# The delta-rule attention's TensorE program without its loop, and the output product in two halves of the array

## The reference: what is computed

```python
k_n = k / (np.linalg.norm(k, axis=-1, keepdims=True) + 1e-06)
state = np.zeros((B, H, D, D), dtype=np.float32)
for t in range(S):
    kt, vt, bt = (k_n[:, :, t], v[:, :, t], beta[:, :, t, None])
    y[:, :, t] = np.einsum('bhd,bhde->bhe', q[:, :, t], state)
    v_old = np.einsum('bhde,bhd->bhe', state, kt)
    state = state + bt[:, :, :, None] * np.einsum('bhd,bhe->bhde', kt, vt - v_old)
```

## Time and profile before

| | us |
|---|---|
| median of three runs | 1100.64 (1093.97, 1100.64, 1100.87) |
| profiled execution: its own time | 1103.74 |
| profiled execution: span | 1102.0 |
| of it, first to last output product of the attention | 66.8 to 396.5 |
| TensorE busy in the span | 967.5 (88%) |
| VectorE | 630.4 (57%) |
| ScalarE | 586.7 (53%) |
| GpSimd | 259.2 (24%) |

### The profile page before, as it was taken

The page is one execution under the profiler, slowest core; times in us unless marked ns, Lnnn a source line. Parts: engine busy times, 40 slices in busy tenths (PEclk is TensorE's granted clock), DMA queues, the critical chain, the costliest instruction groups (busy, mean ns, idle before and its releaser), DMA issues. The chain is left out here.

```text
span 1102.0 us, 25678 instructions
## 1 busy us (share of the span) xinstructions
PE 967.5 (88%) x10563; PEld 673.8 (61%) x10563; DVE 630.4 (57%) x1106; ACT 586.7 (53%) x1141; POOL 259.2 (24%) x303
## 2 busy tenths in 40 slices
PE   1798998989899884069999999999999999999996
PEld 0587887878788752046666667655555555555553
DVE  5678686868678546356665654244444444444442
ACT  2566574747477552346666664354545454454542
POOL 6556463646256111710000000000101001010101
PEclk9989897979799977589999999999999999999998
DMA  6022132312122001774555541000000000000000
GB/s 215 16 81 86 43 102 66 91 55 77 43 69 63 2 1 53 241 252 145 150 155 151 151 155 47 1 1 1 29 1 29 1 1 29 0 29 0 29 1 29
DMA packets 38108, 74.05 MB, mean 67 GB/s; under 512 B 3817, under 2 KB 29553, under 8 KB 38001
## 3 DMA queue, kind: packets, MB, share of 16 engines
q1 hardware_dynamic: 34928, 63.05, 18.5%
q0 software_dynamic: 3072, 9.45, 2.3%
HBM read 63.04 MB, written 9.45 MB: 66 GB/s over the span
## 5 line engine op out<-in xcount | busy, mean ns | idle before, releaser
L1406 PE MATMUL bankH<-rows_or_y,wd 128*128 128x512 f16 (+1 forms) x864 | 201.8, 379 | 1.6 <-PEq L1045 1.6
L1418 PE MATMUL bankO<-wd,gd_hi 128*128 128x384 f16 x768 | 187.4, 326 | 0.6
L1406 PEld LDWEIGHTS bankH<-rows_or_y,wd 128*128 128x128 f16 x864 | 84.5, 98 | 93.5 <-issue 1.7
L665 DVE CAST_PREDICATED merge<-pair_mask,bankA 128x512 f16<-128x512 uint16 x144 | 100.5, 698 | 56.1 <-PE bankA L346 55.9
L1418 PE MATMUL bankO<-wd,gd_lo 128*128 128x384 f16 x384 | 125.2, 326 | 0.0
L534 ACT CAST x_inv<-bankA 128x512 f16<-128x512 f32 x120 | 70.4, 587 | 86.2 <-PE bankA L357 86.2
L1418 PEld LDWEIGHTS bankO<-wd,gd_hi 128*128 128x128 f16 x768 | 74.6, 98 | 62.1 <-DVE gd_lo L1480 2.8
L1503 POOL DMA_INDIRECT out<-o_rows,dest x24 | 25.6, 1069 | 346.7 <-ACT o_rows L1457 290.4
L1473 DVE SCALAR_TENSOR_TENSOR gd<-hd_exp,hd 128x512 f32<-128x512 f32 x96 | 66.5, 692 | 66.8 <-ACT hd_exp L1443 66.8
L1480 DVE SCALAR_TENSOR_TENSOR gd_lo<-gd,gd_hi 128x512 f16<-128x512 f32 x96 | 66.5, 692 | 64.4 <-ACT gd_hi L1451 64.4
L1451 ACT ACTIVATE gd_hi<-gd 128x512 f16<-128x512 f32 x96 | 60.4, 630 | 69.1 <-DVE gd L1473 69.0
(11 more groups left out here) (187 smaller groups left out, 1791.5 us busy)
## 6 DMA issues: line engine op xcount, KB each, us to landing
kq_t<-in_kq_rows SPq DMA_DIRECT2D x24, 512.0 KB, 4.6
stage<-in_moe_w SPq DMA_DIRECT2D x24, 512.0 KB, 3.6
stage<-in_moe_w SPq DMA_DIRECT2D x32, 384.0 KB, 3.6
rows_or_y<-x_sorted SPq DMA_DIRECT2D x12, 385.0 KB, 7.4
k_norm<-in_k_tok SPq DMA_DIRECT2D x24, 192.0 KB, 2.4
v_in<-in_v_tok SPq DMA_DIRECT2D x24, 192.0 KB, 2.4
k_tok<-in_k_tok SPq DMA_DIRECT2D x24, 192.0 KB, 3.5
stage<-in_moe_w_in SPq DMA_DIRECT2D x8, 384.0 KB, 3.2
```

What stands on the lines that cost most here:

```text
L665: nc.vector.copy_predicated(half_cols(merge[:, i], i, False), pair_mask[:, i, :].rearrange("p (n b) -> p n b", b=2 << i).unsqueeze(1) .to_ ...
L1406: last = nc.tensor.matmul(h_bank[f % 4][:, :], wd1[:, a, c, P * f:P * f + P], y_t[:, b, c, bass.ds(blk * NB, NB)], start=c == a == b == 0, ...
L1418: last = nc.tensor.matmul(o_bank[s][:, 0:DM], (g_lo if a else g_hi)[:, f % 4, P * s:P * s + P], wd2[:, b, f, :], start=f == a == b == 0, s ...
```

## The change

TensorE's program in the attention is written out for all 27 bodies (items -3 to 23) by the same `each_item` that the other engines use; the loop and the register-valued waits are gone. And each head's output product becomes two products, of weight columns 0 to 63 and 64 to 127, that write partitions 0 to 63 and 64 to 127 of the output bank. Nothing else moves. Lines behind the removed function have a number lower by 11, from the output product on by 9.

```diff
--- before.py
+++ after.py
@@ -36,24 +36,13 @@
         return Item(self.c, self.b + k)
 
     def exists(self):
-        return not isinstance(self.n, int) or 0 <= self.n < NT
+        return 0 <= self.n < NT
 
 
 def need(eng, sem, value):
 
     if not isinstance(value, int) or value > 0:
         eng.wait_ge(sem, value)
-
-
-def over_items(eng, body):
-
-    for b in range(-GRAM, B):
-        body(Item(0, b))
-    with eng.Fori(1, NCH - 1) as c:
-        for b in range(B):
-            body(Item(c, b))
-    for b in range(B):
-        body(Item(NCH - 1, b))
 
 
 def each_item(first, body):
@@ -423,8 +412,10 @@
 
             def within_chunk(it):
                 for h in range(H):
-                    last = nc.tensor.matmul(out_bank[:, D * h:D * h + D], bt_pt[:, it.b, h, 1, :], u[:, h, :],
-                                            start=False, stop=True, skip_group_check=True)
+                    for f in range(2):
+                        half = slice(DP * f, DP * f + DP)
+                        last = nc.tensor.matmul(out_bank[half, D * h:D * h + D], bt_pt[:, it.b, h, 1, half], u[:, h, :],
+                                                start=False, stop=True, skip_group_check=True)
                 last.then_inc(s_op, 1)
 
             def body(it):
@@ -513,7 +504,7 @@
                         pe.wait_ge(s_yv[5], late.n + 1)
                     merged_y(early, 2)
 
-            over_items(pe, body)
+            each_item(-GRAM, body)
 
         @block.scalar
         def _(act):
```

## The result

The changed kernel takes 1067.38 us (median of 4, 1064.89 to 1069.75), the kernel before 1100.76 us (median of 4): ratio 0.9705, 95% interval 0.9651 to 0.9759, or 33.4 us less. The profiled execution took 1069.75 us, its span is 1068.0 us, 34.0 less than the 1102.0 before.

What follows compares the result with a forecast made beforehand. TensorE was taken as the bound in the attention, lengthened by clock falls and waits at chunk turns. Loop 5.6 plus output product 14.0 made 19.6 us less: 1081 us from a median of 1100.64, range 1071 to 1095.

Steps and rivals of the forecast that it cites:

- The product at full clock: Output product on TensorE in the attention: block from 1.80 to 1.2 us, 0.6 us less per item, 7.2 us in twelve items.
- The law of loads and halves: TensorE weight loads cost 0.84 ns a column; 64-column records take 59 ns, 29.5 if two halves work beside each other.
- A: Rival, output product: no work side by side with 64 columns, 2.1 against 1.80 us a block, 1102 us; 8%.
- C: Rival, output product: load and matmul in turn, 108 ns a record, 3.5 us a block, 1132 us; 4%.
- B: Rival: VectorE becomes the bound in the attention, only 0.3 us an item comes through, 1088 us; 12%.
- D: Rival: TensorE's clock falls more often in the attention; one more fall in each of five chunks gives 1108 us; 5%.
- The loop: Removing TensorE's backward branch, taken three times, gains 1.87 us each, 5.6 us together.
- The holes: TensorE idle behind the branch at items 8, 12 and 16, 6.9 us together; they go, and straight code brings none.
- the rates' wait: At a chunk's turn TensorE waits 2.54 us for VectorE's chain of rates; expected to stay, with the clock's falls.
- the low stretch keeps its length: Items 3, 7, 11, 15 at or near half clock: saved product work counts once at full clock, 2.4 us.
- Rival E: Fewer falls of the clock, or a fall shorter without its hole: 5 to 10 us more gained, 1073 us; 9%.
- the last product: Last item's output product at half clock, on the path to ScalarE's copy: 3.65 to 1.95 us, 1.7 us less.

Runs made afterwards that it cites:

- e5: Changed kernel with the output product whole as before and VectorE's last two rates steps moved to the item's end: 1064.79 us, ratio 0.9665.
- e4: Changed kernel with VectorE's last two steps of the rates moved to the item's end: 1051.95 us, ratio 0.9568.
- the repeat: The kernel before, unchanged, profiled once more: 1099.92 us.
- e2: Changed kernel with the output product whole as before, so only the loop is written out: 1092.62 us, ratio 0.9928.
- e8: Kernel before, with its loop and whole product, only VectorE's last two rates steps moved to the item's end: 1080.96 us, ratio 0.9821.
- e1: Kernel before with its loop, only the output product split into halves: 1091.56 us, ratio 0.9923.
- the two repeats: The kernel before and the changed kernel, each profiled once more: 1099.92 and 1070.53 us.
- e3: Changed kernel with the loops over heads and halves exchanged, so neighbouring products share a half: 1086.29 us, ratio 0.9883.

## Why the prediction was wrong

**The product at full clock: right.** The law of loads and halves gave 29.5 ns a record, 29.6 was measured; leaving the half mode was put at 0.12 to 0.25 us, and 1.07 - 0.95 = 0.12 is what is left. The block was put at 1.2 us with the 0.09 for entering; it is 1.07 and 0.09. An item like item 9 gained 0.63 us (0.6), items 16 to 20 0.33 (0.3): VectorE's identity tile holds the transposes there as foreseen, with waits of up to 0.3 us. All intervals other than the turns gained 9.7 us; the working has 9.9 for them, but part of that agreement is luck. The first interval of a chunk was 12.5 us before and not 12.77, and gained 0.35 us or, in the first chunk, nothing, so the twelve items gave 6.1 us and not 7.2. Items 21 and 22 gave 2.0 in place of 1.2, because the low stretch that lay over item 22 before came only behind it. e5 against e4 gives 12.8 us for the split without any clock, against 14.0. Rivals A and C are out by the block of 1.07 us. B did not come in the changed kernel; D did not come either, the clock over the stage is 0.96.

**The loop: right in what it is, wrong in its price.** The holes are gone, straight code brought none. I priced a branch at 1.87 us by comparing two turns of one trace, one without the branch and one with it. The comparison rested on both having a stretch of 13.6 us. At item 4 that was luck: the repeat has 3.4 us there, and e2, whose program is the same up to that place, 10.2 twice. The same subtraction in the repeat (state changes at 92.41, 147.45 and 208.14 us) gives 60.69 - 55.04 = 5.65 us. e8 against e5, where nothing else lets the clock fall, gives 5.4 us a branch, with holes of 3 us and a low stretch behind each. A branch has no one price: with the rates' wait in place, taking out the loop gained 2.7 us a branch beside the whole product (before to e2) and 8.1 beside the halves (e1 to the changed kernel).

**The step that failed** is "the low stretch keeps its length", under which I counted saved work in items 3, 7, 11 and 15 once, 2.4 us, and 5.6 us for the holes: 8.0 us at the four turns. They gave 24.3 (16.4 between the two repeats). The stretches shrank from 58 us together (41 in the repeat) to 20.5. Runs show two causes that need each other. Without the hole they end earlier: at the three turns with a branch 44 and 38 us in the two traces of the kernel before, 24 in both with the whole product written out. With the halves they end earlier still (20.5 us at all four turns, 17.1 and 13.7 in e3, where the block is no shorter, against 34.1), but in the loop (e1) the hole brings the clock down again (41 us). Hence 9.1 us for the split alone, 8.1 for the straight program alone, and 33.4 for both. Put as a path over e2, the loop gave 8.1 us (5.6 in the sum) and the split 25.2 (14.0 in the sum), of which e4 and e5 put 12.4 down to the clock.

**Rival E** ("a fall is shorter without the hole in it", 1073, 9%) named half of the mechanism and was given too little: I had the price of one fall, 5.3 us, and the span of the runs, but no question of what the changed work would do to four falls at once. The range's lower end counted one fall less.

**At the end** of the attention the last product ran partly at full clock (its group is 1.52 us long), which gave 2.6 in place of 1.7 us. The later stages, with the same program, took 2.2 us more, with 54.6 us of low clock in the routing against 51.2.

**Open:** why the halves let the clock come back sooner. e3 rules out the block's length; what else in the program decides it (the number of records, the half mode itself, where the groups fall in time) was not isolated.

## What to carry to other kernels

Products with f32 weights of 128 columns and few moved columns were bound by the weight load here (112 ns a record, 107 of them for the columns' load by the line's own durations); split into halves that alternate, a block took 1.07 instead of 1.80 us with 48 columns moved and 0.81 instead of 1.04 with 96, and nothing was gained where neighbours shared a half (48 columns). Look for short waits behind which the clock falls, and price them as wait plus stretch: moving two steps of 0.19 us on VectorE away from a busy GpSimd gained 15 us on top of this change, more than the split product's own 12.8. Do not price a stretch of low clock from one execution, and where two parts of a change both touch it, expect them not to add up.

## What the runs showed of the hardware

- Two halves of the array work side by side for f32 products that use all 128 rows: 29.6 ns a record with a load of 64 columns (54 ns by the prediction's law of loads). In e3, where neighbours share a half, the record costs 53 ns. The Trainium skill, in "TensorE: Matmul & The Clock Gate", Part 3, has loads overlap only where the row group differs; no row group differs here, and the trace decides against it.
- A taken backward branch on TensorE left a hole of 2.2 to 2.4 us in the kernel before and of 2.75 to 3.5 us in e8, and was enough to bring the clock from 1.00 to 0.50 (e8). The Trainium skill, "Runtime: NRT & Kernel Launch", Instruction fetch mechanics, says that a taken branch to code outside the two pages that the engine holds must fetch the target before going on. The trace agrees: a 16 KB packet of the instruction queue lies in each hole of e8. No run varied what the branch has to fetch, so that the fetch is all of the hole is not shown.
- A VectorE step of 32 elements a row took 1.88 us beside GpSimd's 1024-element product (kernel before), ending with it, and 0.19 us away from it (e4).
